# Attention output and state update of a decayed linear attention in 64-column tiles of TensorE (one Trainium2 core)

## The reference

```python
# r, k, v, w: batch 4, heads 8, tokens 768, channels 48;  u: 8 x 48
state = zeros((B, H, D, D))
for t in range(S):
    cur = einsum('bhd,bhe->bhde', u[None] * kt, vt)
    y[:, :, t] = einsum('bhd,bhde->bhe', rt, state + cur)
    state = wt[:, :, :, None] * state + einsum('bhd,bhe->bhde', kt, vt)
# 3072 tokens x 384
h = x @ w_in            # 384 x 2048
g = where(h >= 1, h, where(h <= -1, 0, (h + 1) ** 2 / 4))
x2 = g @ w_out
out = (silu(x2 @ w_gate) * (x2 @ w_val)) @ w_out2    # width 1536
```

## Time and profile before

| | us |
|---|---|
| median of 3 runs | 1050.95 |
| their range | 1050.66 to 1052.82 |
| the profiled execution, whole | 1050.49 |
| its span in the profile | 1048.6 |
| TensorE busy, matmul / weight load | 1004.0 / 990.1 |
| DVE busy / ACT busy / POOL busy | 555.8 / 394.5 / 133.6 |

### The profile page before, as it was taken

One profiled execution on the slowest core, in us unless ns is written; L12 is line 12 of the kernel. 1 busy time (PEld: TensorE's weight loads), 2 busy tenths in 40 slices (PEclk: granted clock), 3 DMA queues, 4 the chain that ended last, 5 costly groups with the idle time before them and its releaser, 6 DMA issues.

```text
span 1048.6 us, 15818 instructions
## 1 busy us (share of the span) xinstructions
PE 1004.0 (96%) x6162; PEld 990.1 (94%) x6162; DVE 555.8 (53%) x958; ACT 394.5 (38%) x799; POOL 133.6 (13%) x90
## 2 busy tenths in 40 slices
PE   1689999999999999999999999999999999999997
PEld 0679999999999999999999999999999999999997
DVE  7866584774947759477444443343434343433332
ACT  3445344453454535544366532222222222222221
POOL 4650030110301203002026320000000000000000
PEclk9989999999999999999999999999999999999999
DMA  6450140400503105030033211001010101010000
GB/s 225 149 181 27 30 142 1 144 27 3 168 1 132 39 2 170 1 121 24 1 121 98 91 53 46 2 1 46 1 45 0 45 0 45 0 45 0 23 1 25
DMA packets 23199, 59.63 MB, mean 57 GB/s; under 512 B 2657, under 2 KB 11489, under 8 KB 23137
## 3 DMA queue, kind: packets, MB, share of 16 engines
q1 hardware_dynamic: 23136, 58.79, 17.1%
HBM read 49.34 MB, written 9.44 MB: 56 GB/s over the span
## 4 chain that ended last, share of the span: by engine, by line
PE 92%; DVE 4%; issue 1%; ACT 1%; DMA 1%; SPq 0%; DVEq 0%; ACTq 0%
PE bank L1039 47%; PE bank L1063 34%; PE bank L1108 4%; PE bank L1089 2%; PE bank L1104 2%; PE bank L1098 1%; PE bank L1082 1%; PE bank L1113 1%; DVE w_window L835 1%; DVE r_by_channel L860 1%; DVE k_by_channel L852 1%; DVE suf L830 1%; DVE w_by_channel L843 0%; DMA w_by_channel<-in_w_channel 0%; DMA ring<-in_w_out 0%
## 5 line engine op out<-in xcount | busy, mean ns | idle before, releaser
L690 ACT ACTIVATE ghi<-gate 128x384 fp32r<-128x384 f32 x224 | 117.9, 526 | 256.7 <-PE bank L1063 111.3
L916 DVE TENSOR_TENSOR glo<-gate,ghi 128x384 fp32r<-128x384 f32 x224 | 136.5, 610 | 115.8 <-ACT ghi L690 113.4
L933 DVE TENSOR_TENSOR gate<-bank,gate 128x384 f32<-128x384 f32 x96 | 53.6, 558 | 221.6 <-ACT gate L794 221.6
L1039 PE MATMUL bank<-xlo,w2gv_ahi 128*128 128x384 f32 x480 | 162.1, 338 | 0.0
L1039 PE MATMUL bank<-xhi,w2gv_alo 128*128 128x384 f32 x480 | 162.1, 338 | 0.0
L1039 PE MATMUL bank<-xhi,w2gv_ahi 128*128 128x384 f32 x480 | 162.1, 338 | 0.0
L1063 PE MATMUL bank<-ghi,w1ohi 128*128 128x384 f32 x384 | 136.9, 357 | 3.1 <-DVE glo L916 3.1
L794 ACT ACTIVATE gate<-bank 128x384 f32<-128x384 f32 x96 | 47.3, 493 | 234.1 <-PE bank L1039 234.1
L1039 PE MATMUL bank<-xhi,w1ihi 128*128 128x384 f32 x384 | 130.7, 340 | 1.3 <-DVE xlo L911 1.3
L1039 PE MATMUL bank<-xlo,w1ihi 128*128 128x384 f32 x384 | 130.5, 340 | 0.0
L1039 PE MATMUL bank<-xhi,w1ilo 128*128 128x384 f32 x384 | 130.4, 339 | 0.0
(11 more groups left out here) (81 smaller groups left out, 1607.9 us busy)
## 6 DMA issues: line engine op xcount, KB each, us to landing
w_by_channel<-in_w_channel SPq DMA_DIRECT2D x16, 339.5 KB, 3.8
k_by_channel<-in_k_channel SPq DMA_DIRECT2D x16, 336.0 KB, 4.8
r_by_channel<-in_r_channel SPq DMA_DIRECT2D x16, 336.0 KB, 5.5
ring<-in_w_out SPq DMA_DIRECT2D x28, 192.0 KB, 2.7
r_k_diag<-in_r_token SPq DMA_DIRECT2D x8, 576.0 KB, 7.0
k_by_token<-in_k_token SPq DMA_DIRECT2D x8, 576.0 KB, 8.0
v_by_token<-in_v_token SPq DMA_DIRECT2D x8, 576.0 KB, 9.1
x_t<-ring SPq DMA_DIRECT2D x8, 576.0 KB, 3.3
```

The source lines that it names most:

```text
L690: e.activation(ghi[j % 2][:, :], gate[j % 2][:, :], ACT.Copy).then_inc(M["hi", ph], 1)
L916: e.tensor_tensor(glo[j % 2][:, :], gate[j % 2][:, :], ghi[j % 2][:, :].bitcast(F32), ALU.subtract)\
L933: e.tensor_tensor(q, hid[j % 2][:, 0:T], q, ALU.mult).then_inc(M["t", 2], 1)
L1039: m = e.matmul(out, w_of(a, k), x_of(b_, k), start=start and i == 0, stop=stop and i == total - 1)
```

## The change

Y: each matmul is split into two, one for the tokens 0 to 63 of the window and one for 64 to 127 (`HALVES`). The weights have 64 columns in place of 128, the moving columns stay as they are, and the result goes to the upper or the lower 64 PSUM partitions, that is to one of two column tiles of the array. There are twice as many matmuls.

ST: each head has a matmul of its own, with 64 (even head) or 48 (odd head) weight columns, in its own column tile, and 48 moving columns. The blocks between heads are no longer formed; a pair's two blocks lie above one another in PSUM and in the state `st`, which shrinks from 96 to 48 columns per pair. `sbar` keeps its block-diagonal form for Y, so `decay_state` becomes two DVE operations of 48 partitions x 192, and the counts of `st_dec` double.

```diff
-        st, _ = place("state", [PR, NPAIR, 2 * D], F32)
+        st, _ = place("state", [PR, NPAIR, D], F32)
...
                 if w == 0 and parity == 0:
-                    e.memset(sbar[:, :, :], 0.0).then_inc(st_dec, 1)
+                    e.memset(sbar[:, :, :], 0.0).then_inc(st_dec, 2)
                     return
-                wt = wtot[parity][:, :, w:w + 1].to_broadcast([PR, NPAIR, 2 * D])
-                e.tensor_tensor(sbar[:, :, :], st[:, :, :], wt, ALU.mult).then_inc(st_dec, 1)
+                for i in range(2):
+                    r0, c0 = 64 * i, D * i
+                    rows = slice(r0, r0 + D)
+                    wt = wtot[parity][rows, :, w:w + 1].to_broadcast([D, NPAIR, D])
+                    e.tensor_tensor(sbar[rows, :, c0:c0 + D], st[rows, :, :], wt, ALU.mult).then_inc(st_dec, 1)
...
-                    e.wait_ge(st_dec, g * NW + (w + 1))
+                    e.wait_ge(st_dec, g * (2 * NW) + (2 * w + 2))
                     n_pair = state_pairs(w, parity)
                     for i in range(2):
                         r0, c0 = 64 * i, D * i
-                        blk = (slice(r0, r0 + D), slice(0, n_pair), slice(c0, c0 + D))
-                        ps = src[r0:r0 + D, 0:n_pair * 2 * D].rearrange("p (a c) -> p a c", a=n_pair)[:, :, c0:c0 + D]
-                        e.tensor_tensor(st[blk], ps, sbar[blk], ALU.add).then_inc(st_out, 1)
+                        rows, pairs = slice(r0, r0 + D), slice(0, n_pair)
+                        ps = src[rows, 0:n_pair * D].rearrange("p (a c) -> p a c", a=n_pair)
+                        e.tensor_tensor(st[rows, pairs, :], ps, sbar[rows, pairs, c0:c0 + D], ALU.add).then_inc(st_out, 1)
...
+            HALVES = (slice(0, WIN // 2), slice(WIN // 2, WIN))
...
-                    for p in range(state_pairs(w, parity)):
-                        m = e.matmul(out[0:PR, p * 2 * D:(p + 1) * 2 * D], ktk[w % 2][:, p * PR:(p + 1) * PR],
-                                     vn[:, w, p * 2 * D:(p + 1) * 2 * D], start=True, stop=True)
+                    for h in range(2 * state_pairs(w, parity)):
+                        p, r = h // 2, slice(0, 64) if h % 2 == 0 else slice(64, PR)
+                        m = e.matmul(out[r, p * D:(p + 1) * D], ktk[w % 2][:, p * PR:(p + 1) * PR][:, r],
+                                     vn[:, w, h * D:(h + 1) * D], start=True, stop=True)
                 elif kind == "Y":
-                    e.wait_ge(st_dec, g * NW + (w + 1))
+                    e.wait_ge(st_dec, g * (2 * NW) + (2 * w + 2))
                     row_start = w == 0 and parity == 0
                     for p in range(0 if row_start else NPAIR):
-                        e.matmul(out[:, p * 2 * D:(p + 1) * 2 * D], rd[:, p, cols(w)], sbar[:, p, :],
-                                 start=(p == 0), stop=False, skip_group_check=True)
+                        for t in HALVES:
+                            e.matmul(out[t, p * 2 * D:(p + 1) * 2 * D], rd[:, p, cols(w)][:, t], sbar[:, p, :],
+                                     start=(p == 0), stop=False, skip_group_check=True)
                     e.wait_ge(at_out, g * (2 * NW) + (2 * w + 2))
                     for h in range(H):
-                        m = e.matmul(out[:, h * D:(h + 1) * D], att[h % 2][:, h // 2, :], vn[:, w, h * D:(h + 1) * D],
-                                     start=(row_start and h == 0), stop=(h == H - 1), skip_group_check=True)
+                        for t in HALVES:
+                            m = e.matmul(out[t, h * D:(h + 1) * D], att[h % 2][:, h // 2, t],
+                                         vn[:, w, h * D:(h + 1) * D], start=(row_start and h == 0),
+                                         stop=(h == H - 1), skip_group_check=True)
```

## The result

The changed kernel took 1037.71 us (median of 4 runs, 1034.98 to 1037.86) against 1051.38 for the kernel before: a ratio of 0.9862 (95% interval 0.9842 to 0.9882). The forecast was 1037.5. In two later sessions, on other chips, the same kernel came out at 0.9875 (0.986 to 0.989) and 0.9860 (0.9842 to 0.9878).

What follows compares the result with a forecast made beforehand. TensorE, busy 96% of the span, was taken as the bound. Y's savings of 13.7 and 1.6 us less ST's losses of 0.5 and 1.2 made 13.6 us, taking 1050.95 us to the stated 1037.5; range 1028 to 1072.

Steps and rivals of the forecast that it cites:

- TensorE's slots set the end: From 130 to 525 us TensorE is busy 394.78 of 395.00 us, so a microsecond saved there shortens the kernel by one.
- Side by side: Two column tiles in Y and ST load and stream at once, 55 ns a pair: 1037.5 us, chance 0.50.
- second rival: Loads of two column tiles go one after the other, as they read the same partitions: +16.7 us, 1067.5, chance 0.27.
- fourth rival: A column tile's load no longer hides behind the matmul ahead of it: +13.9 us, 1065, chance 0.10.
- third rival: Partial overlap, or something else such as instruction issue, holds pairs near 80 ns: 1049 us, chance 0.13.
- 82 ns a pair: In Y's r-times-state part, streaming 96 moving columns sets a pair's price, at most 82 ns by AT's pace.
- For `att` I took 55: In Y's att-times-v part, a pair costs one 64-column load, half of a 128-column one: 55 ns.
- The fee: Entering and leaving the tiled form costs each of 42 Y and ST blocks 0.40 us, 16.8 us in all.
- The other edits: `decay_state` as two DVE operations takes 0.65 us for 0.55, 20 times, hidden; ST's additions and the smaller memset cost nothing.
- The start: Half 0's shorter Y on the chain only waits for a load of weights: nothing counted, 1 us for the range.

Runs made afterwards that it cites:

- joined kernel: The changed kernel with each ST moved directly ahead of the Y of its window: 1028.67 us, 0.9783.
- control: The kernel before, without tiles, with only the step order altered so that each ST stands directly ahead of its Y: 1049.13 us, 0.9982.
- quarters: The changed kernel with Y in four column tiles of 32 tokens: 1032.16 us, 0.9821.
- halves in turn: The changed kernel with Y's matmuls reordered, in each part first all of tokens 0 to 63, then all of 64 to 127: 1054.93 us, 1.0034.

## Why the prediction was right

**That TensorE's slots set the end**, and a microsecond less there is one less in all: right. The slots stayed full in the windows. The price of a block as read from the timeline, times its count, gave the measured time in the joined kernel (0.34 x 21 = 7.1 us worked out, some 7 measured once the control's 2 are off) and in the quarters (1.94 to 1.69 us a Y, 0.25 x 21 = 5.3 worked out, about 5 measured).

**Side by side**, the step with half the chance: right. Two loads of column tiles begin together although they read the same partitions. The experiment with the halves in turn shows that it is this, and not the narrower loads, that makes the gain: without neighbours in different tiles the same matmuls are slower than the kernel before. So a loss such as the second rival had can be had, 3.6 us and not its 16.7, but it comes from the order of the matmuls and not from the partitions that the tiles share. The fourth rival, a load that no longer hides, would have given pairs of (55 + 41) ns in a tile; a pair in two tiles with `att` took 59 in all, and a record alone in its tile 58. The Trainium skill's rule that a load overlaps with matmuls in flight only when the row group differs ("TensorE: Matmul & The Clock Gate", Part 3, The mechanism) doesn't hold here: all rows were shared, and loads of both tiles, 0.08 us apart, ran beside matmuls 0.25 us long. The third rival's pairs near 80 ns came only where 96 columns stream; for `att` they were 59, and the issue of instructions as the bound is refuted by the quarters.

**The terms.** For 96 moving columns I took 82 ns a pair, from AT's stream: the loads came 82 ns apart, and with quarters still did, so this one is the stream, at the slower of the two bounds that I had for it, 43 and 82. For `att` I took 55; it is 58 to 59. The fee I took as 0.40; a Y of 1.94 us less 8 x 0.082 and 16 x 0.059 leaves 0.34, and an ST 0.80 - 8 x 0.057 = 0.34. The two errors cancel in a Y, whose 1.94 us were met; that is luck. For ST a loss of 0.03 was forecast and a gain of 0.01 came, for one pair 0.51 forecast and 0.46 measured: due 0.32 after the XT at 117.43, ended 0.17 ahead of 118.38.

```profile
117.43 0.49 PE L1121 MATMUL bank<-cst,x_by_token 128*128 128x128 f32 x3
117.85 0.32 PE L1103 MATMUL bank<-v_by_token,k_token 128*64 128x48 f32 x4
118.09 0.45 PE L1067 MATMUL bank<-ghi,w1ohi 128*128 128x384 f32 x1
118.38 0.34 PE L1067 MATMUL bank<-glo,w1ohi 128*128 128x384 f32 x1
```

With a row-beginning Y of 1.27 for 1.82 the measured prices give 18 x 0.76 + 3 x 0.55 + 17 x 0.01 - 4 x 0.24 = 14.5 us, against 13.6 forecast.

**The other edits.** `decay_state` on DVE went from the earlier trace rows's 17.6 us to 19.4, 1.8 more where 20 x 0.1 = 2 were forecast, and hidden as forecast: the waits of PE on `att` and on the decayed state, 2.3 and 1.9 us (1.4 each before), lie in the start. The groups of DVE in the changed kernel:

```profile
L885 DVE TENSOR_TENSOR state_decayed<-state,w_window 48x192 f32<-48x192 f32 x40 | 19.4, 485 | 0.6
```

**The start.** Nothing was forecast from it, though half 0 has 3 Y of its own. The first L1043 starts at 63.65 us where L1039 started at 63.56, and TensorE's wait for `xn` grew from the earlier trace rows's 7.8 us to 12.4: the shorter Y became a longer wait. By the wait for `glo` the two traces are level: the first L1067 behind it starts at 79.63 us, L1063 started at 79.64.

```profile
PE bank L1121 <- DVE x_by_token L911: 12.4, 2, 7.9
...
PE bank L1115 <- DVE att L897: 2.3, 2, 2.0
PE bank L1110 <- DVE state_decayed L885: 1.9, 1, 1.9
```

**What the forecast did not have.** The profiled execution's span fell by 12.5 us, not by 14.5. In it the granted clock was 0.66 from 80 to 85 us, right after TensorE had waited 2.9 us for `glo`, and it was 1.00 in the same stretch before. The L1043 ahead of the next KT starts at 84.27 us where L1039 started at 82.73, so the fall cost 1.5 us. 14.5 less 1.5 are 13.0; the other 0.5 us stay open. That fall is not the change's: the profiles of the same kernel in the two later sessions show 1.00 there and spans of 1034.1 and 1034.5, 14.5 and 14.1 below the 1048.6 of before, and the control without tiles shows the fall. That the median was met to 0.2 us is luck too: the gain in the slots was 0.9 us larger than forecast and the fall went the other way in this profile, and by the medians of the three sessions the gain is 13.7, 14.2 and 15.2 us.

## What to carry to other kernels

Where small matmuls cost the load of their weights and not their stream, as the starts in the timeline tell, cut the weights' columns into column tiles and put matmuls of different tiles next to each other in program order; the order is worth as much as the tiles. Count the fee of entering and leaving the tiled form, about 0.34 us here: a block of 0.8 us gains nothing, and blocks of one tile width placed back to back pay once. Narrow the tiles until the stream is the bound, in all steps of the block alike.

## What the hardware showed that was not expected

- Loads of column tiles, all from the same 112 or 128 partitions, begin together: two of 64 columns, and four of 32, each 7 ns behind the one before it.
- The array reaches ahead over the seam between two tiles: with the halves in turn, up to four loads of the two halves were in flight where one half followed the other, and this halved the expected loss, 17 in place of 33 us.
- Eight instructions (four loads, four matmuls) went out in 45 ns.
- A change from 64 to 32 tile columns, without an untiled matmul between, cost 0.13 us, as the difference of two blocks' lengths.
- In the start, the granted clock of the earlier trace rows reads 1.00 from 40 to 55 us, but L1108's 16 records there took 3.67 us and start 213 ns apart, not 108, as at the lower of the clock's two levels, 1.2 GHz. In that stretch the durations were to be trusted and not the clock. The changed kernel's profile does read 0.50 there:

```profile
40.00:55.00 15.00, 10.60 (x115) 8.95 (x117) 14.51 (x26) 5.04 (x11) 8.22 (x8) 0.50 0.42 126
```
